# Fourier mixing on Trainium2: the sequence step with one source per residue instead of two

## The reference

```python
X = np.fft.fft(x, axis=1)
X = np.fft.fft(X, axis=2)
u = x + np.real(X)
un = (u - mu) / np.sqrt(var + 1e-06)      # over the channels
ch = np.maximum(un @ w_ch1, 0.0) @ w_ch2  # hidden width 1280
return u + ch
```

## Time and profile before

| | us |
|---|---|
| median of 3 runs | 381.36 (380.81 to 381.92) |
| the profiled execution | 380.41 |
| its span | 378.6 |
| PE matmul busy | 369.9 (98%), 2411 matmuls |
| DVE, ACT, POOL busy | 189.5, 149.9, 110.9 |

### The profile page before, as it was taken

One profiled execution on the slowest core, in us unless ns is written; L12 is line 12 of the kernel. 1 busy time (PEld: TensorE's weight loads), 2 busy tenths in 40 slices (PEclk: granted clock), 3 DMA queues, 4 the chain that ended last, 5 costly groups with the idle time before them and its releaser, 6 DMA issues.

```text
span 378.6 us, 6173 instructions
## 1 busy us (share of the span) xinstructions
PE 369.9 (98%) x2411; PEld 357.5 (94%) x2411; DVE 189.5 (50%) x391; ACT 149.9 (40%) x307; POOL 110.9 (29%) x107
## 2 busy tenths in 40 slices
PE   8998999999999999999999999999999999999997
PEld 3788998999999999999999999999999999999996
DVE  7888665555253252055931585448924484341421
ACT  5678798568342241012550144514433201330310
POOL 6258788548132000000193000723570000000000
PEclk9999999999999999999999999999999999999999
DMA  7978899532130000022022000523040001001000
GB/s 153 249 190 218 262 304 254 144 105 93 42 108 17 19 0 0 19 84 88 3 87 71 0 2 6 221 71 137 3 138 19 2 1 36 17 2 36 16 19 35
DMA packets 17024, 30.95 MB, mean 82 GB/s; under 512 B 2452, under 2 KB 7700, under 8 KB 16996
## 3 DMA queue, kind: packets, MB, share of 16 engines
q1 hardware_dynamic: 16084, 29.64, 27.1%
q0 software_dynamic: 192, 0.66, 0.6%
q10 hardware_dynamic: 720, 0.27, 0.3%
HBM read 26.60 MB, written 3.96 MB: 81 GB/s over the span
## 4 chain that ended last, share of the span: by engine, by line
PE 84%; DVE 3%; ACT 3%; POOL 1%; issue 1%; ACTq 0%; DVEq 0%; POOLq 0%
PE ps L641 30%; PE ps L618 23%; PE ps L621 4%; PE ps L620 4%; PE ps L500 4%; PE ps L727 4%; PE ps L476 3%; PE ps L576 3%; PE ps L554 2%; PE ps L745 2%; PE ps L594 2%; PE ps L485 2%; POOL m_lo L1421 1%; PE ps L510 1%; PE ps L462 1%
## 5 line engine op out<-in xcount | busy, mean ns | idle before, releaser
L927 ACT ACTIVATE h_hi<-ps 128x384 fp32r<-128x384 f32 x88 | 43.3, 492 | 115.9 <-PE ps L621 115.9
L1172 DVE SCALAR_TENSOR_TENSOR h_lo<-ps,h_hi 128x384 fp32r<-128x384 f32 x88 | 48.5, 555 | 55.4 <-ACT h_hi L927 54.9
L1178 DVE TENSOR_TENSOR xt<-ps,xt 128x320 f32<-128x320 f32 x24 | 11.8, 491 | 69.1 <-PE ps L641 69.1
L641 PE MATMUL ps<-ch_hi,h_hi 128*128 128x320 f32 x144 | 45.5, 316 | 0.0
L641 PE MATMUL ps<-ch_hi,h_lo 128*128 128x320 f32 x144 | 44.5, 309 | 0.0
L641 PE MATMUL ps<-ch_lo,h_hi 128*128 128x320 f32 x144 | 44.5, 309 | 0.0
L641 PE MATMUL ps<-m_hi,h_hi 128*128 128x320 f32 x120 | 37.4, 312 | 0.6 <-POOL m_lo L1421 0.6
L641 PE MATMUL ps<-m_hi,h_lo 128*128 128x320 f32 x120 | 37.1, 309 | 0.0
L641 PE MATMUL ps<-m_lo,h_hi 128*128 128x320 f32 x120 | 37.1, 309 | 0.0
L618 PE MATMUL ps<-uT_hi,ch_hi 128*128 128x384 f32 x96 | 33.0, 344 | 0.5 <-DVE h_lo L1172 0.5
L1421 POOL TENSOR_TENSOR m_lo<-m_raw,m_hi 128x640 fp32r<-128x640 f32 x11 | 18.1, 1669 | 50.9 <-ACT m_hi L794 50.9
(11 more groups left out here) (164 smaller groups left out, 882.7 us busy)
## 6 DMA issues: line engine op xcount, KB each, us to landing
kq<-in_kq SPq DMA_DIRECT2D x24, 192.0 KB, 4.9
ch_raw<-in_ch SPq DMA_DIRECT2D x11, 384.0 KB, 5.3
vk<-in_vk SPq DMA_DIRECT2D x12, 328.0 KB, 4.6
m_raw<-in_m SPq DMA_DIRECT2D x11, 320.0 KB, 4.2
og<-in_o SPq DMA_DIRECT2D x12, 160.0 KB, 4.7
x_scratch<-xt SPq DMA_DIRECT2D x12, 160.0 KB, 1.8
out<-xt SPq DMA_DIRECT2D x12, 160.0 KB, 1.8
tok_raw<-in_tok SPq DMA_DIRECT2D x4, 384.0 KB, 7.0
```

Of the source, the lines that this page charges most:

```text
L641: mm = pe.matmul(bank, h[hx][:, f, i * P:(i + 1) * P], w[wx][:, f], start=(f == 0 and hx == 0 and wx == 0), stop=(f == FCH[k] - 1 and hx = ...
L927: act.activation(h[0][:, f], h_bank(k, f), ACT.Relu).then_inc(hhi_done, 1)
L1172: dve.scalar_tensor_tensor(out=h[1][:, f], in0=h_bank(k, f), scalar=0.0, in1=f32(h[0][:, f]), op0=ALU.max, op1=ALU.subtract).then_inc(hlo_ ...
L1178: dve.tensor_tensor(xt[:, tile], o_bank(n), xt[:, tile], ALU.add).then_inc(o_done, 1)
```

## The change

**What is computed.** Both sources of a residue pair are combined before the matmul. With the sequence constants rewritten (`dft_constants`), each q has one source: rows from `fold`, to which a reversed copy of other rows (partition p takes row 128 - p) is added. The reversal goes through memory: DVE forms the rows to send (step 10, four operations into two tiles of `un`), SP stores them to `back_scratch` (`store_back`, after `store_first` for the row p = 0), POOL loads them in reversed order by an indirect DMA (`load_back`), and DVE adds them (step 11). `seq` shrinks from 1536 to 1024 columns, `eo` and `em` from 768 to 512 elements of a partition, and `fold` has no zeroed gap.

**What moves.** m goes 1, 2, 0 (`ORDER`), and the channel step has m outside and q inside. The reload of x no longer waits for `folded` but for step 9. Three `h_lo` of block 3 stand among the six `mixed(0)` (`MIXED_LO`). The deviations and `normalize(0)` come two f later. The fifth piece of the layer 2 weights is split in block 4 (`SPLIT_M2`). The high parts of batch 1's folds move from the end of block 4 to f = 3, 4, 5 of block 5, and step 11 of batch 1 is in f = 1 of block 5; that of batch 0 behind the second output tile of block 2.

```diff
+PLACE = [2, 0, 3, 1]
+ORDER = (1, 2, 0)
+BACK_AFTER = 1
+MIXED_LO = (1, 3, 4)
+SPLIT_M2 = (3, 5, 6, 8, 9)
+NTH = [3, 1, 2]
-FOLD_STEPS = 18
+FOLD_STEPS = 24
...
+            def store_back(b):
+                sp.wait_ge(fold_step, FOLD_STEPS * b + 22)
+                sp.dma_start(back_d[b][0:P], un[:, b * NC:b * NC + 2].rearrange("p a d -> p (a d)")).then_inc(st_back[b], 16)
+            def store_first(b):
+                sp.wait_ge(fold_step, FOLD_STEPS * b + 18)
+                first = back_d[b][P:P + 1].rearrange("o (r d) -> o r d", r=2)
+                for place, cols in ((2, slice(0, EVEN)), (4, slice(EVEN, DM))):
+                    sp.dma_start(first[:, :, cols], fold[0:1, place:place + 2, cols]).then_inc(st_back[b], 16)
...
+                    store_first(0)
                     reload(0)
+                    store_back(0)
...
             def sequence_dft(b):
-                for m in range(NM):
+                for m in ORDER:
...
                     for q in range(NQ):
-                        half = q // 2
-                        sources = ((2 + 2 * half, 0), (3 + 2 * half, P)) if q % 2 == 0 else ((half, 2 * P),)
                         if m == 0:
-                            todo = [(em[:, y, sine].rearrange("p h k -> p (h k)"), sine, first, wx)
-                                    for sine in range(2) for y, first in sources for wx in range(2)]
+                            todo = [(em[:, PLACE[q], sine].rearrange("p h k -> p (h k)"), sine, wx)
+                                    for sine in range(2) for wx in range(2)]
                         else:
-                            todo = [(eo[yx][:, y, m - 1], m - 1, first, wx)
-                                    for y, first in sources for yx, wx in ((0, 0), (0, 1), (1, 0))]
+                            todo = [(eo[yx][:, PLACE[q], m - 1], m - 1, wx) for yx, wx in ((0, 0), (0, 1), (1, 0))]
...
             def channel_dft(b):
-                order = [(q, m) for m2 in ((0, 1), (2,)) for q in (0, 1) for m in m2]
-                for q, m in order + [(q, m) for q in range(2, NQ) for m in range(NM)]:
+                for q, m in [(q, m) for m in ORDER for q in range(NQ)]:
...
-                    if k == 3 and f == 1:
+                    if k == 3 and f == 3:
                         deviations(0)
-                    if k == NBLK and f in (4, 6, 8, 9):
-                        split_hi(N_M1 + (4, 6, 8, 9).index(f))
+                    if k == NBLK and f in SPLIT_M2:
+                        split_hi(N_M1 + SPLIT_M2.index(f))
...
+                    if k == NBLK + 1 and f in (3, 4, 5):
+                        folds_hi(1, ORDER[f - 3:f - 2])
...
                 elif step == 7:
                     ready(14)
-                    dve.memset(fold[:, :, 161:ODD_TAIL], 0.0).then_inc(fold_step, 1)
...
+                elif step == 10:
                     ready(18)
+                    for r, sign in ((0, -1.0), (1, 1.0)):
+                        stt(sent[:, r, even], F[:, 4 + r, even], 1.5 * sign, F[:, 2 + r, even])
+                        stt(sent[:, r, odd], F[:, 4 + r, odd], -0.5 * sign, F[:, 2 + r, odd])
+                elif step == 11:
+                    dve.wait_ge(ld_back[b], 16)
+                    dve.wait_ge(st_back[b], 48)
+                    stt(F[:, 2, even], back[:, 0, even], 0.5, F[:, 2, even])
+                    stt(F[:, 3, even], back[:, 1, even], -0.5, F[:, 3, even])
+                    dve.tensor_tensor(F[:, 4:6, odd], F[:, 4:6, odd], back[:, :, odd], ALU.add).then_inc(folded, 1)
...
-                    if k == 2 and f < 10:
+                    if k == 2 and f < 11:
                         fold_tokens(0, f)
-                    if k == 3 and 2 <= f < 2 + NC:
-                        normalize(0, f - 2)
+                    if k == 3 and 4 <= f < 4 + NC:
+                        normalize(0, f - 4)
+                    if k == NBLK + 1 and f == 1:
+                        fold_tokens(1, 11)
...
                 if k == NBLK:
-                    for step in (7, 8, 9):
+                    for step in (7, 8, 9, 10):
                         fold_tokens(1, step)
...
                         mixed(0, jp)
+                        if jp in MIXED_LO:
+                            hidden_lo(3, MIXED_LO.index(jp))
...
+            def load_back(b):
+                pool.wait_ge(st_back[b], 48)
+                pool.indirect_dma_start(un[:, b * NC + 2:b * NC + 4].rearrange("p a d -> p (a d)"), None, back_d[b],
+                                        bass.IndirectOffsetOnAxis(ap=turned_rows[:, 2:3], axis=0)
+                                        ).then_inc(ld_back[b], 16)
...
+            pool.wait_ge(tm2_done, NT)
+            pool.memset(f32(em[:, :, :, :, :].rearrange("p y s h k -> p (y s h k)")), 0.0).then_inc(em_zero, 1)
+            pool.wait_ge(fold_step, 22)
+            for n in range(N_ATT, N_ATT + 2):
+                split_lo(n)
+            load_back(0)
+            for n in range(N_ATT + 2, N_DFT):
+                split_lo(n)
             folds_lo(0)
             reload_turned(0)
             for n in range(N_DFT, len(PIECES)):
                 split_lo(n)
+            load_back(1)
             folds_lo(1)
             reload_turned(1)
```

More of the change, by code:

```diff
@@ L65, in dft_constants @@
 def dft_constants():
[L67 to L74, removed]
+    n = np.arange(P)[:, None]
+    banks = [[], []]
+    for r in (1, 0, 2, 3):
+        theta = 2 * np.pi * (r + NC * np.arange(P))[None, :] / S
+        if r % 3 == 0:
+            banks[0] += [np.cos(theta * n)]
+            banks[1] += [-np.sin(theta * n)]
+        else:
+            c, d = np.cos(np.pi * r / 3), np.sin(np.pi * r / 3)
+            half = (np.cos(theta * n) - c / d * np.sin(theta * n) + np.sin(theta * (P - n)) / d) / 2
+            even, odd = half.copy(), -d * half
+            even[0] = 1 / (1 + c)
+            odd[0] = -d / 2
+            banks[0] += [even]
+            banks[1] += [odd]
+    seq = np.concatenate(banks[0] + banks[1], axis=1)
     angle = 2 * np.pi * np.outer(np.arange(DM), np.arange(DM)) / DM
@@ L88 @@
 L_ATT = len(LOADS)
-LOADS += [("seq", n * 768, 768) for n in range(2)] + [("chan", 0, 2 * DMX), ("chan", 2 * DMX, DMX)]
+LOADS += [("seq", n * 512, 512) for n in range(2)] + [("chan", 0, 2 * DMX), ("chan", 2 * DMX, DMX)]
 L_DFT = len(LOADS)
@@ L215, in build @@
     ea_d = nc.dram_tensor("ea_scratch", [NC, H, CH], F32, kind="Internal").ap()
+    back_d = [nc.dram_tensor(f"back_scratch{b}", [P + 1, 2 * DM], F32, kind="Internal").ap() for b in range(B)]
     x2_d = [nc.dram_tensor(f"x2_scratch{b}", [S, DM], F32, kind="Internal").ap() for b in range(B)]
@@ L318, in lo_split, with folded_count, sources, pairs_of @@
         eng.wait_ge(wlo_done, n + 1)
-    def tail_cols(t):
-        return t[:, :, FOLD_PART[0]].rearrange("p c (s k) -> p c s k", s=2)
+    def folded_count(b, m):
+        return 4 * b + (4, 1, 2)[m]
+    def sources(m, cols):
+        if m == 2:
+            return fold[:, :, cols].rearrange("p (g two) k -> p g two k", two=2)[:, 0:3:2]
+        return fold[:, 0:NQ, cols].rearrange("p (g two) k -> p g two k", two=2)
+    def pairs_of(t):
+        return t.rearrange("p (g two) k -> p g two k", two=2)
     def f32(ap):
@@ L709, in sequence_dft @@
             def sequence_dft(b):
[L710 to L713 removed]
+                for m in ORDER:
+                    pe.wait_ge(eohi_done, folded_count(b, m))
+                    pe.wait_ge(eolo_done, folded_count(b, m))
+                    if b == 1 and m == ORDER[0]:
                         pe.wait_ge(Ulo_done, NM)
@@ L1185, in output @@
                         fold_tokens(1, i)
+                    if k == 2 and i == BACK_AFTER:
+                        fold_tokens(0, 11)
             dve.wait_ge(ld_gates2, 16)
@@ L1223, in fold_tokens @@
                 xb = xt[:, b * NC:(b + 1) * NC]
-                pm = fold[:, :, 0:DM]
+                pm, F = fold[:, :, :], fold[:, :, :]
+                sent = un[:, b * NC:b * NC + 2]
+                back = un[:, b * NC + 2:b * NC + 4]
                 before = b * FOLD_STEPS
+                even, odd = slice(0, EVEN), slice(EVEN, DM)
                 def ready(n):
@@ L1533 @@
         "seq": seq, "chan": chan, "ident": np.eye(P, dtype=np.float32),
-        "turned": np.array([[NC * (P - 1 - p) + j for j in (4, 5)] for p in range(P)], np.int32), "roles": roles, "sel": sel.reshape(P, 2 * P),
+        "turned": np.array([[NC * (P - 1 - p) + j for j in (4, 5)] + [P - p] for p in range(P)], np.int32), "roles": roles, "sel": sel.reshape(P, 2 * P),
         "mask": np.where(later, np.float32(NEG), np.float32(0)),
```

120 lines of the change are left out of this document (63 added, 57 removed).

## The result

The changed kernel takes **375.31 us** (374.62 to 376.1, 4 runs) against 381.09 (4 runs of before): ratio 0.9847, 95% interval 0.982 to 0.9873, so 5.8 us faster. A later, separate measurement gave 375.54 against 381.14. The forecast was 375.7.

What follows compares the result with a forecast made beforehand. TensorE, its matmuls busy 98% of the span at full clock, was taken as the bound. Gains 4.43 + 0.5 + 0.4 + 0.3 = 5.6 from 380.41 gave 374.8; with 0.95 for the median, 375.7 us; range 374.0 to 378.4.

Steps and rivals of the forecast that it cites:

- Matmuls removed: Sequence step, both batches: 40 matmuls instead of 60 per batch at 0.1108 us each, 4.43 us gained in both.
- Channel step by groups: Channel step, both batches: the new order ends the waiting for the third part of U, 0.5 us gained in both.
- Interleaving: Block 3's first layer at batch 0's end: three h_lo among the mixings cut the loss from 0.78 to about 0.4, gain 0.4.
- Last weights: Block 4's layer 2: the 0.74 us stop for the fifth weight split goes, less a new output tile wait; gain 0.3.
- the pile-up: Rival 2, VectorE in block 4: steps 4, 5, 6 meet splits, ninth h_lo late; 376.9 or 378.1 us, chance 0.13.
- The wait for the output tile: Block 4's layer 2, third tile: step 10 delays VectorE's output tile; wait of 0.25 to 0.65 us, taken as 0.45.
- Round trip: Scratch memory store and reversed load, batch 0 and batch 1: all hidden behind other work, cost 0.
- the third rival: Round trip lands late; in batch 1 TensorE stops once store and load exceed 9.7 us; up to 382.3, chance 0.05.

Runs made afterwards that it cites:

- the old nesting: Changed kernel with the channel step in the old order (q = 0 and 1 with the first two column groups, then the third; then q = 2, 3): 376.68 us.
- the longer step 10: Changed kernel with four more operations of step 10's size behind batch 1's step 10, their result unused: 376.22 us, 0.7 above its partner, the changed kernel's 375.54.
- the late store: Changed kernel with batch 1's store to scratch memory issued behind block 4's third output store: 377.61 us, 2.1 above the changed kernel's 375.54.
- no interleaving: Changed kernel with no h_lo of block 3 among batch 0's six mixings (MIXED_LO empty): 378.38 us, 3.1 slower than the changed kernel.
- the late step 11: Changed kernel with batch 0's step 11 behind the third output tile of block 2 instead of the second: 384.89 us, ratio 1.0097 to the kernel before.

## Why the forecast was right, step by step

**Matmuls removed**, 4.43 forecast: 4.48 in the stretches, and 4.48 again when 40 were put back. Right, and the row (0.111 us each) holds against the 81 ns that the Trainium skill gives ("TensorE: Matmul & The Clock Gate", section "Back-to-back issue gap").

**Channel step by groups**, 0.5 forecast: 0.31. The waits went, but each channel step still takes 0.10 above 32 x 0.1466: the first matmul is followed after 0.21 instead of 0.147, and the others, with 322 columns, stand 0.148 apart. I had counted both as waiting. Beside the tails-last order the edit is worth more than either number: with the old nesting each batch lost 0.55 there.

**Interleaving**, 0.4 forecast: 0.24. The clock of events was right to 0.1 (third mixing's add ends 12.27 us after the sequence step's start, forecast 12.2), but behind the gap TensorE needs 0.1 to be at its distance again. What failed here is the comparison, not the arithmetic: I priced the edit against the kernel before, where the gap was 0.66. Beside the shorter steps the same missing edit costs 2.2 to 2.5, because TensorE arrives 2.4 us earlier and VectorE's chain only 0.5, and 3.7 to 3.9 where the clock falls as well. The forecast did not say this.

**Last weights**, 0.3 forecast: 0.72. The stall, 0.86 of layer 2's 14.13 against the undisturbed 13.27, went entirely (2.8 us after layer 2's start the ninth h_lo starts in both kernels, so the pile-up is neither worse nor better than before). The wait for the output tile that I put at 0.45 cost 0.14. The mis-sized term: I took 0.45 between a wait of 0.25 and one of 0.65, the second for other collisions on VectorE, and there were none more; and the tile ends 8.86 us after layer 2's start, not 9.04, because taking the memset out of the folds saved 0.47 (steps 7 and 8 up to the copy took 2.67 before and take 2.20) where I had counted 0.29. That the tile was so near is shown by the longer step 10. The same run answers the forecast's remark that step 10 costs only where a split is still running: GpSimd's last split had ended at 268.1 in the changed kernel, step 10 starts at 272.85, and the added operations still came back nearly in full.

**Round trip**, 0: right, with less to spare than I counted on. In batch 0 the load lands by about 201, 2 us before VectorE wants it at 202.87 (3.2 forecast); in batch 1 VectorE waits 0.23 and TensorE nothing. SyncE's timeline, batch 0's store:

```profile
191.59 0.33 SPq L422 DMA_DIRECT2D back_scratch<-un  x1
```
GpSimd's timeline, the load that waits for it:

```profile
196.74 1.12 POOL L1525 DMA_INDIRECT un<-back_scratch,turned_rows  x1 [2.54 <-DMA back_scratch<-un]
```
The same of batch 1, SyncE's store:

```profile
274.50 0.42 SPq L422 DMA_DIRECT2D back_scratch<-un  x1
```
GpSimd's load:

```profile
279.61 0.96 POOL L1525 DMA_INDIRECT un<-back_scratch,turned_rows  x1 [11.53 <-DMA back_scratch<-un]
```
And VectorE's step 11, which reads the landed rows:

```profile
283.27 0.57 DVE L1280 SCALAR_TENSOR_TENSOR fold<-un,fold 128x161 f32<-128x161 f32 x2 [0.23 <-DMA un<-back_scratch,turned_rows]
```

In both batches 5.1 us pass from the issue of the store, behind the reload, to the release of GpSimd (3.5 and 3.9 were forecast), and the load of batch 1 lands 3.7 after its issue starts. From the end of step 10 (273.88) to the landing it is 9.4 us; the forecast had 8.5, of the 10.7 after which TensorE would feel it (the 9.7 of the third rival and 1.0 for GpSimd's issue). That leaves 1.3, and the late store shows 1.1, where I had counted on 2.2: the slower rival was nearer than I took it to be.

**The sum.** -0.19 and -0.16 from the second and third term, +0.42 from the fourth and 0.05 from the first add to 0.1: 5.75 instead of 5.6. That the sum is this near is in part luck, as the errors of three terms cancel; the first term, four fifths of the sum, is not luck. The median lay 0.7 above the profiled execution of before, not 0.95 as I took it from three runs; with the 0.1 of the sum this puts the forecast 0.4 above the measurement.

## What to carry to other kernels

When one engine is the bound and a step on it is shortened, every wait behind it has to be looked at again with that engine earlier: an edit that looked worth 0.2 us against the kernel before was worth at least 2.2 after. A trip through memory is free as long as the consumer stands behind work that is there anyway; where that is, decides more than how long the trip is (with step 11 of batch 0 behind one more output tile the kernel was 9.3 us slower). And times by stretch, from TensorE's starts, repeat to 0.01 to 0.03 us where the whole time varies by 2.

## What the runs showed of the hardware

- Gaps of TensorE (idle time, as in the brackets of the lines above) and the granted clock: after 0.5 to 0.8 us (before, and the longer step 10) and after 1.6 (the late store) it stayed at 2.4 GHz. After 2.4 (no interleaving) it went to 1.2 GHz 1.5 us later, for 3.2 us, in the profiled execution, and fell in four of nine executions. After 3.6 (the late step 11) it went there 0.9 later, for 10.2, and fell in five of five. In the profiled executions TensorE had no other gap near these. The cost of the fall, 1.5 and 4.9 us, was over half of the gap's own length in the one case and more than it in the other. Why the one lasted three times as long as the other was not settled.
- At half clock the distance between matmuls was 0.32 for 384 columns (0.1735 at full), 0.27 for 322 (0.147) and 0.213 for 128 (0.111).
